# Last products on rows in block order, loaded inside the last expert block, and one-tile blocks with the rows stationary

## What is computed

```python
def reference(**kw):                          # cut to what matters, all fp32
    # 1. attention, 2 x 8 heads x 768 x 64: a window of +-15 keys and, beside it,
    #    24 summaries (max of k, mean of v over blocks of 32 keys), one softmax
    x = attn(q, k, v)                         # as rows [1536 tokens, 512]
    # 2. expert layer: each token goes to one of 8 experts
    logits = x @ w_gate
    expert_idx = argmax(logits, axis=1)
    gate_w = softmax(logits)[token, expert_idx]
    for e in range(8):                        # tokens of expert e
        out[mask] = gate_w[mask, None] * (relu(x[mask] @ w1[e]) @ w2[e])   # 512 -> 1024 -> 512
    # 3. dense layer, leaky relu
    h = out @ w_in                            # 512 -> 2048
    return maximum(0.01 * h, h) @ w_out       # 2048 -> 512
```

## Time and profile before

| | |
|---|---|
| median of 3 runs | 562.81 us (562.48 to 565.88) |
| the profiled execution | 563.63 us, of which the span from first to last instruction 561.9 us |
| mean granted TensorE clock | 0.987 of full |
| TensorE busy | 530.7 us, 94% of the span |
| VectorE / ScalarE / GpSimd busy | 53% / 48% / 14% |
| chain of work that ended last | TensorE 80%, VectorE 5%, ScalarE 5%, DMA 4% |
| HBM | 68.3 MB read, 11.3 MB written |

### The profile page before, as it was taken

One profiled execution on the slowest core, in us unless ns is written; L12 is line 12 of the kernel. 1 busy time (PEld: TensorE's weight loads), 2 busy tenths in 40 slices (PEclk: granted clock), 3 DMA queues, 4 the chain that ended last, 5 costly groups with the idle time before them and its releaser, 6 DMA issues.

```text
span 561.9 us, 9620 instructions
## 1 busy us (share of the span) xinstructions
PE 530.7 (94%) x3309; PEld 439.5 (78%) x3310; DVE 299.6 (53%) x575; ACT 267.7 (48%) x569; POOL 81.1 (14%) x123
## 2 busy tenths in 40 slices
PE   4899998979999999998869999999999999999997
PEld 3477777877888888898758888888888888888885
DVE  2678787774345245187715624754723763742631
ACT  4388778524344244378615525623633641642520
POOL 6127503014301310233200000000000000000000
PEclk9999999998999999999879999999999999999999
DMA  9999569028604524357770243144064052340001
GB/s 214 216 239 239 140 201 324 20 86 326 224 22 169 207 73 168 120 190 255 274 262 0 89 164 123 49 152 174 0 224 149 0 187 67 119 149 0 0 19 56
DMA packets 77964, 79.96 MB, mean 142 GB/s; under 512 B 45552, under 2 KB 47600, under 8 KB 77936
## 3 DMA queue, kind: packets, MB, share of 16 engines
q1 hardware_dynamic: 73168, 66.48, 38.7%
q0 software_dynamic: 3040, 9.96, 5.4%
q10 hardware_dynamic: 1728, 3.15, 1.5%
HBM read 68.30 MB, written 11.27 MB: 142 GB/s over the span
## 4 chain that ended last, share of the span: by engine, by line
PE 80%; DVE 5%; ACT 5%; DMA 4%; issue 3%; POOL 1%; SPq 0%; POOLq 0%; ACTq 0%; DVEq 0%
PE psum L1364 12%; PE psum L1365 12%; PE psum L1366 12%; PE psum L1382 11%; PE psum L1383 11%; PE psum L1384 11%; PE psum L1291 2%; PE psum L1224 2%; ACT p_sb L671 1%; PE psum L1279 1%; DMA y_rows<-y_sb,home_idx 1%; PE psum L1215 1%; PE psum L1180 1%; PE psum L1262 1%; PE psum L1199 1%
## 5 line engine op out<-in xcount | busy, mean ns | idle before, releaser
L1364 PE MATMUL psum<-xT_hi,w_hi 128*128 128x512 f32 (+2 forms) x352 | 130.2, 370 | 2.2 <-DVE w_lo L891 1.4
L1365 PE MATMUL psum<-xT_lo,w_hi 128*128 128x512 f32 (+2 forms) x352 | 129.0, 367 | 0.0
L1366 PE MATMUL psum<-xT_hi,w_lo 128*128 128x512 f32 (+2 forms) x352 | 128.9, 366 | 0.0
L1382 PE MATMUL psum<-w_hi,h_hi 128*128 128x512 f32 x296 | 116.9, 395 | 0.1
L1383 PE MATMUL psum<-w_lo,h_hi 128*128 128x512 f32 x296 | 116.0, 392 | 0.0
L1384 PE MATMUL psum<-w_hi,h_lo 128*128 128x512 f32 x296 | 115.8, 391 | 0.0
L891 DVE TENSOR_TENSOR w_lo<-w_raw,w_hi 128x512 fp32r<-128x512 f32 x88 | 57.0, 687 | 61.9 <-ACT w_hi L700 61.9
L1364 PEld LDWEIGHTS psum<-xT_hi,w_hi 128*128 128x128 f32 x352 | 66.7, 190 | 13.2 <-DVE xT_lo L901 2.8
L1366 PEld LDWEIGHTS psum<-xT_hi,w_lo 128*128 128x128 f32 x352 | 66.7, 190 | 10.2
L1365 PEld LDWEIGHTS psum<-xT_lo,w_hi 128*128 128x128 f32 x352 | 66.8, 190 | 10.0
L747 ACT ACTIVATE h_small<-psum 128x512 f32<-128x512 f32 x48 | 28.7, 598 | 89.8 <-PE psum L1366 89.8
(11 more groups left out here) (182 smaller groups left out, 535.6 us busy)
## 6 DMA issues: line engine op xcount, KB each, us to landing
w_raw<-in_moe_w_in SPq DMA_DIRECT2D x12, 1024.0 KB, 6.5
w_raw<-in_moe_w_out SPq DMA_DIRECT2D x6, 2048.0 KB, 8.5
w_raw<-in_moe_w SPq DMA_DIRECT2D x10, 1024.0 KB, 6.2
w_raw<-in_moe_w SPq DMA_DIRECT2D x5, 2048.0 KB, 8.3
q_nat<-in_q SPq DMA_DIRECT2D x12, 256.0 KB, 4.6
x_rows<-x_cur ACTq DMA_DIRECT2D x12, 256.0 KB, 3.8
x_rows_sb<-y_rows SPq DMA_DIRECT2D x12, 256.0 KB, 8.3
result<-y_sb SPq DMA_DIRECT2D x12, 256.0 KB, 2.0
```

Source lines behind the costliest of these rows:

```text
L1364: mm(h, w1_hi[:, c, cols], xT_hi[:, c, 0:n], start=(c == 0), stop=False)
L1365: mm(h, w1_hi[:, c, cols], xT_lo[:, c, 0:n], start=False, stop=False)
L1366: last = mm(h, w1_lo[:, c, cols], xT_hi[:, c, 0:n], start=False, stop=(c == KD - 1))
L1382: mm(y_ps[s % 2], h_hi[:, c, rows], w2_hi[:, c, :], start=(c == 0), stop=False)
```

## The change

1. The expert layer's results go to `y_dram` not at their token's row but at a "seat": block 1's rows first, then the later blocks' without the padding between them, and block 0's at the end. A column is added to `y_sb`, `x_rows` and `y_dram` (513 values a row) that carries the token's number. Padding rows go behind the 1536 real ones.
2. The first 512 seats are full when block 3 is stored. SP loads them inside block 4, and TensorE transposes them in two halves around the middle and the end of tile 0 of block 4's second product. The fill matmuls and the extra transposes go.
3. The gates are stored to DRAM once and fetched for each group of 512 by token number; each output tile is scattered by GpSimd to its tokens' rows.
4. A block of one tile runs its first product the other way round: the 128 rows stationary, 512 columns of w1 streaming, 2 x 4 x 3 = 24 matmuls. The hidden rows pass the relu, are transposed (8 transposes) and split after that.
5. In block 0: ScalarE makes the last w1 high parts together, GpSimd the four low parts of the upper half; VectorE makes slots, marks and plan in another order, with three w2 splits behind them; TensorE's inversion also waits for the plan. SP loads block 1's weights ahead of its loop.

The core of the diff (declarations, constants and repeated slices left out):

```diff
@@ SP
-            with sp.Fori(0, MAXB) as j:
+            next_e = sp.value_load(plan[0:1, 1:2], min_val=0, max_val=E - 1)
+            sp.wait_ge(w1_lo_ready, KF)
+            load_w1(next_e)
+            sp.wait_ge(w2_lo_ready, KF)
+            load_w2(next_e)
+            with sp.Fori(1, MAXB) as j:
...
                     with sp.If(n_blocks < j + 2):
-                        load_half(0, j + 1)
...
+                        load_half_w1(0, j + 1)
+                        sp.wait_ge(rows_transposed, KD * (j + 1))
+                        sp.sem_inc(sp_wait_over, 1)
+                        sp.wait_ge(y_stored, 16 * (SUB * j - (SUB - SUB0)))
+                        sp.sem_inc(sp_wait_over, 1)
+                        load_rows(0)
+                        load_half_w2(0, j + 1)
...
             sp.wait_ge(y_stored, 16 * (SUB * n_later + SUB0))
-            load_rows(0)
-            sp.sem_inc(y_out_free, 1)
...
-                for s in range(SUB):
-                    sp.wait_ge(y_ready, (u + 1) * SUB + s + 1)
-                    sp.dma_start(out[ds(g * ROWS + s * P, P), :], y_sb[:, s, :]).then_inc(out_stored, 16)
@@ GpSimd
+            pool.wait_ge(w1_lo_ready, KD)
+            for c in range(KD):
+                part = slice(F // 2, F)
+                pool.wait_ge(w1_hi_ready, KD + c + 1)
+                tt(w1_lo[:, c, part], w1_raw[:, c, part], w1_hi[:, c, part].bitcast(F32),
+                   ALU.subtract).then_inc(w1_lo_ready, 1)
...
+            def keep_ids(g):
+                for s in range(SUB):
+                    pool.wait_ge(rows_loaded[s], 16 * (g + 1))
+                nc.gpsimd.tensor_copy(out_idx[:, g, :], x_rows[:, :, DM].bitcast(I32)).then_inc(out_idx_ready, 1)
+                pool.wait_ge(out_idx_ready, g + 1)
+            def gather_gates(g):
+                if g:
+                    pool.wait_ge(y_ready, SUB * (n_blocks + HALVES * g))
+                    pool.sem_inc(out_wait_over, 1)
+                for s in range(SUB):
+                    pool.indirect_dma_start(
+                        out=row_gate[:, s:s + 1], out_offset=None, in_=gate_dram[:, :],
+                        in_offset=bass.IndirectOffsetOnAxis(ap=out_idx[:, g, s:s + 1].bitcast(U32), axis=0),
+                    ).then_inc(row_gate_ready, 16)
...
+            for g in range(GROUPS):
+                if g + 1 < GROUPS:
+                    keep_ids(g + 1)
+                for s in range(SUB):
+                    pool.wait_ge(y_ready, SUB * (n_blocks + HALVES * g + 1) + s + 1)
+                    pool.sem_inc(out_wait_over, 1)
+                    pool.indirect_dma_start(
+                        out=out[:, :], out_offset=bass.IndirectOffsetOnAxis(ap=out_idx[:, g, s:s + 1].bitcast(U32), axis=0),
+                        in_=y_sb[:, s, 0:DM], in_offset=None,
+                    ).then_inc(out_stored, 16)
+                if g + 1 < GROUPS:
+                    gather_gates(g + 1)
@@ ScalarE
+            def relu_tile(u):
+                for f in range(KD):
+                    split_w2(u, f)
+                for i in range(2):
+                    act.wait_ge(h_done, KF * u + 2 * i + 2)
+                    nc.scalar.activation(h_full[:, i, :], h_ps[i], ACT.Relu).then_inc(h_hi_ready, 2)
+                    for f in range(KD + 2 * i, KD + 2 * i + 2):
+                        split_w2(u, f)
+            def round_tile(u):
+                for i in range(2):
+                    act.wait_ge(h_done, KF * u + KD + 2 * i + 2)
+                    nc.scalar.copy(h_hi[:, KD * i:KD * i + KD, 0:P],
+                                   h_ps[2 + i].rearrange("p (f t) -> p f t", t=P)).then_inc(h_hi_ready, 2)
...
+                    used = act.value_load(used_tiles[0:1, ds(j, 1)], min_val=1, max_val=SUB)
@@ VectorE, block 0
             for f in range(KF):
                 rest_of_relu(0, f, ROWS0)
-                split_w2(0, f)
-                if W1_LEFT + f < KF:
-                    split_w1(0, W1_LEFT + f)
+                if f < 5:
+                    split_w2(0, f)
...
                 if f == 5:
-                    later_experts()
+                    dve.wait_ge(places_done, 2)
                     later_slots()
-                if f == 6:
                     slot_parts(T)
                     hot_tiles(T, LATER_TILES)
-            hot_rows(T)
+                if f == 6:
+                    hot_rows(T)
+                    later_experts()
+            for f in range(5, KF):
+                split_w2(0, f)
+            shift_logits()
+            later_tables()
             keep_gates()
-            later_tables()
@@ TensorE
-            def keep_busy(count):
-            def transpose_loaded_rows():
+            def first_of_tile(u, x):
+                for i in range(2):
+                    cols = slice(i * ROWS, (i + 1) * ROWS)
+                    for c in range(KD):
+                        pe.wait_ge(w1_lo_ready, 8 * u + KD * i + c + 1)
+                        if i == 0:
+                            pe.wait_ge(xT_lo_ready, KD * x + c + 1)
+                        mm(h_ps[i], xT_hi[:, c, 0:P], w1_hi[:, c, cols], start=(c == 0), stop=False)
+                        mm(h_ps[i], xT_hi[:, c, 0:P], w1_lo[:, c, cols], start=False, stop=False)
+                        last = mm(h_ps[i], xT_lo[:, c, 0:P], w1_hi[:, c, cols], start=False, stop=(c == KD - 1))
+                    last.then_inc(h_done, 2)
+            def transpose_hidden(u):
+                for i in range(2):
+                    pe.wait_ge(h_hi_ready, KF * u + 2 * i + 2)
+                    for f in range(KF // 2):
+                        last = nc.tensor.transpose(h_ps[2 + i][:, f * P:(f + 1) * P], h_full[:, i, f * P:(f + 1) * P], ident[:])
+                    last.then_inc(h_done, 2)
...
+            pe.wait_ge(experts_ready, 2)
             invert(inv_ps, T, LATER_TILES)
...
                     with pe.If(j + 1 < n_blocks):
                         transpose_rows(j + 1, rows_gathered, j + 2, 0, 2)
-                    second_product(j, 0, 1)
+                    with pe.If(used < 2):
+                        transpose_hidden(j)
+                    second_part(j, 0, 0, KF // 2)
+                    with pe.If(n_blocks < j + 2):
+                        transpose_rows(j + 1, rows_loaded, 1, 0, 2, 0)
+                    second_part(j, 0, KF // 2, KF)
```

More of the change, by code:

```diff
@@ L125, in build @@
         spare_row = keep("spare_row", [P, SLOT_TILES])
+        first_seat = keep("first_seat", [P, SUB0])
+        later_seat = keep("later_seat", [P, MAXB - 1, SUB])
+        padding = keep("padding", [E, P])
+        shift = keep("shift", [P, MAXB - 1, 1])
+        behind_pad = keep("behind_pad", [P, MAXB - 1, E])
         start_rows = keep("start_rows", [E, T, E], BF16)
@@ L159, in build @@
         used_f = keep("used_f", [1, MAXB - 1, 1])
-        ends = keep("ends", [1, 1, E])
-        behind = keep("behind", [1, MAXB - 1, E])
+        behind = keep("behind", [P, MAXB - 1, E])
         expert_f = keep("expert_f", [1, MAXB - 1, 1])
@@ L324, in build @@
         y_out_free = sem("y_out_free")
+        out_wait_over = sem("out_wait_over")
         def piece(m):
@@ L638, in _ @@
                     scatter(j)
+            def keep_ids(g):
[12 more added lines that the diff above has]
+                    ).then_inc(row_gate_ready, 16)
+            keep_ids(0)
+            pool.wait_ge(gate_stored, 16)
+            gather_gates(0)
+            n_later = pool.value_load(plan[0:1, MAXB + 1:MAXB + 2], min_val=1, max_val=MAXB - 1)
+            pool.wait_ge(y_stored, 16 * (SUB * n_later + SUB0))
+            pool.sem_inc(y_out_free, 1)
+            for g in range(GROUPS):
+                if g + 1 < GROUPS:
+                    keep_ids(g + 1)
+                for s in range(SUB):
+                    pool.wait_ge(y_ready, SUB * (n_blocks + HALVES * g + 1) + s + 1)
[6 more added lines that the diff above has]
+                    gather_gates(g + 1)
+                pool.wait_ge(out_stored, 16 * SUB * (g + 1))
+                pool.sem_inc(y_out_free, 1)
         @block.scalar
@@ L760, in second_product @@
                         split_w1(next_u, 2 * s + 1)
+                    if rows is not None:
+                        split_rows(rows, 0, 2)
                     if evacuate:
@@ L992, in count_blocks @@
                 last.then_inc(blocks_ready, 1)
+                dve.wait_ge(blocks_ready, 1)
+                stt(out=padding[:], in0=blocks[:], scalar=-float(ROWS), in1=total_ps,
+                    op0=ALU.mult, op1=ALU.add).then_inc(padding_ready, 1)
             def later_experts():
                 dve.wait_ge(places_done, 2)
-                chain(tt(behind[:], ends_ps.to_broadcast([1, MAXB - 1, E]),
-                         iota_tile[0:1, 0:MAXB - 1].unsqueeze(2).to_broadcast([1, MAXB - 1, E]), ALU.is_le))
-                chain(nc.vector.reduce_sum(expert_f[:, :, 0], behind[:], AX_X))
```

(22 more changed lines are left out.)

146 lines of the change are left out of this document (86 added, 60 removed).

## The result

The changed kernel takes 576.84 us in the median (575.67 to 578.67, 4 runs), the kernel before 563.22 beside it (4 runs). The ratio is 1.0211, 95% interval 1.0161 to 1.0261. The forecast was 558.3, range 551.5 to 565: wrong in sign. The profiled execution took 575.67, span 573.9, which is 12.0 us over the span before.

What follows compares the result with a forecast made beforehand. TensorE never waits in the long middle; gains lie in one-tile blocks and the open seam. Terms 2.0 + 3.7 - 2.1 - 9.95 + 1.8 = -4.55 take 563.63 to 559.1, less 0.8 for the median: 558.3, range 551.5 to 565.

Steps and rivals of the forecast that it cites:

- Block 3's gather: In block 3, gather of block 4's rows shares DMA with the earlier w2 load: +0.6 us, bounds 0 to +2.
- The rule on completion: A DMA's completion follows its engine's earlier writes; so block 4's gather, issued ahead of w2, would take 0.6 us less.
- Row length: Stored and loaded rows grow from 2048 to 2052 B; no cost taken.
- the rule on splitting: Runs off a 256 B multiple fetch up to 8 beats more on 64; under 1 us at the seam.
- a slow seam: Rival: row loads (+5.5) and scatter (+2.3) at the seam are slow, time 566.1; chance 0.13.
- The clock in block 3: In block 3, TensorE's idle of 7 us brings a clock dip: +1.2 us, bounds 0 to 1.7.
- Seam: From block 4's second product to the last stage's second hidden tile: 16.65 us, before 26.6, so -9.95.
- Tail: At the end, last rows leave by GpSimd's indirect DMA instead of SP's plain one: +1.8 us, bounds +0.7 to +3.
- the front: To the start of block 1: gather +0.5 and clock dip +1.6, +2.0 us, bounds -1 to +3.
- block 4: To its second product, ScalarE sets the pace: 11.4 us instead of 13.5, -2.1, bounds -4 and 0.
- the two full blocks: Middle blocks change nothing: products stand back to back, with the splits beside them.
- the last stage: After the second hidden tile, 266 us of the same dense work; its feeding has several us of slack per group.

Runs made afterwards that it cites:

- e1: Changed kernel, but SP loads the next block's second weights only after the block's last row gather has landed; ratio 1.0117.
- e3: Changed kernel, with one-tile blocks running the first product in the old 256-column form; ratio 1.0063.
- e6: Changed kernel with x_rows_sb and y_sb allocated at 528 columns a row in SBUF instead of 513; ratio 1.0207.
- e12: Kernel before, with y_rows in DRAM and y_sb at 513 columns, all 513 scattered and 512 loaded; ratio 1.0043.
- e9: Changed kernel with rows of 528 columns (2112 bytes) in DRAM and SBUF, the id written sixteen times behind each row; ratio 1.0143.
- e10: Changed kernel with 2112-byte rows and the next w2 load held until the last gather has landed; ratio 1.0100.
- e2: Changed kernel, with TensorE's block loop over the 4 later blocks this input has instead of all 10 possible; ratio 1.0154.
- e5: Kernel before, with GpSimd made to wait until the last output tile but one group is stored, then write one element; ratio 1.0080.
- e13: Changed kernel, with the wait for the last group's output stores moved from GpSimd to SP; ratio 1.0169.
- e7: Kernel before, with x_rows_sb alone allocated at 513 columns a row instead of 512; ratio 1.0132.
- e15: Kernel before with x_rows_sb of 513 columns, allocated behind xT_hi and h_small so that these do not move; ratio 1.0025.
- e4: Changed kernel with block 0 in its old order and no splits on GpSimd; ratio 1.0191.
- e8: Changed kernel with 528-column SBUF pitch, one-tile blocks in the 256-column form and TensorE's loop ended after block 4; ratio 1.0021.
- e14: Changed kernel with 2112-byte rows, 256-column form, TensorE's loop ended after block 4, and the last store wait moved to SP; ratio 0.9966.
- e11: Changed kernel with 2112-byte rows, one-tile blocks in the 256-column form and TensorE's loop ended after block 4; ratio 0.9997.

## Why the prediction was wrong

- **Block 3's gather, +0.6 with bounds 0 to 2, is the step that failed**: the wait ended 18.2 us after the block's first product instead of 12.25, so +6.0: 0.45 by later issue, the rest by the fourth gather's landing, 10.2 us for 4.7. I saw that the gather would be what is late, and that the w2 load moves up beside it (forecast 244.4, issued at 245.54), but had no row for a load issued behind a gather and took 0.6 us for it. e1 shows 2.9 us of it, the rows' length is 1.6 to 1.9, and 1.1 stays open. The rule on completion, by which the gather would not suffer, speaks only of the order in which completions are written; the same page of the Trainium skill (DMA: Bandwidth & Descriptors, Queues, rings and completion order) also says that each DMA engine takes turns between its queues packet by packet. The trace agrees as far as a load issued later does slow a gather issued earlier (10.2 against 7.3 us, e1); the third gather, in flight beside the same load, took 7.6 against 7.4.
- **Row length, priced at nothing.** I looked for its cost in the odd rows' own transfers, as the rule on splitting in the Trainium skill (DMA: Bandwidth & Descriptors, How a descriptor splits into AXI transactions) has it, and named a slow seam as the rival. (Its 8 beats on 64 are an eighth, not the seventh that I wrote.) The row loads at the seam took 4.1 us in the median against 3.5 before, but with the same rows 3.4 in e3 and 3.3 in e6, and e12, which reads 2048 bytes out of each row of 2052, took 3.5: nothing pins the 0.6 us on the rows. The pairs around e9 show it elsewhere, on gathers issued behind the scatter: 1.6 to 1.9 us in block 3.
- **The clock in block 3**, +1.2: from the gather's end to block 4's first product took 13.0 us, before 7.4; +5.6 where +3.1 was forecast (1.9 and 1.2). The second product started at half speed and reached full speed at 264.3, and cost 2.0 us more than before, the rows' transposes 0.9; the hidden transposes and their handover took 2.6. In e10, with 8.2 us of waiting, the second product ran at full speed and the same stretch took 11.1 (254.88 to 265.95). But the length of the wait alone does not set the dip: behind 10.7 us in e9 the second product ran at full speed (5.6 us), behind 9.8 in e1 it took 7.3.
- **Seam, -9.95**: came out at -5.35. Its first links were right: SP's loads went out 7.2 us after the last scatter's issue (forecast 6.9), SP loaded rows 1.2 us after block 4's second product began (1.75). Wrong were the loop's exit (3.0 us more between the transposes and the product, which e2 takes away, for 0.75 of waiting on VectorE), the row loads (6.45 us for 5.3; the rows of before give 5.1) and the clock in the first hidden tile (4.4 for 3.45). The exit stood in the timeline before, 2.25 us put down to "issue"; I took it away together with the fill products behind it.
- **Tail, +1.8 with bounds 0.7 to 3**: +6.2. I counted two ways to store a tile. They came to +1.1 (4.83 us from the last product to GpSimd's closing, before 3.75 to SyncE's at 561.67). What I left out is that the engine that waits for the last store must also close: the other 5.1. e5 gives 3.0 us for that alone, e13 gets 1.9 back; why the closing is 5.14 us here and not 3.2 is open.
- **Right**: the front (+1.0, in +2.0 with bounds -1 to 3, the gather and the dip as described), block 4 (-1.4 for -2.1, ScalarE setting the pace), the two full blocks, and the last stage, whose feeding cost nothing (261.78 against 261.77). The front's number is partly luck: in single traces block 3 starts at 236.1 to 240.5 us with the old front (e5, e7, e12, e15) and at 237.4 to 242.4 with the new, so that 1 us can't be told there, and e4's ratio can't tell it either.

The terms that failed are 7.9, 4.6 and 4.4 us. Block order and early rows save nearly what they were counted for once the loop's exit is gone: 9.0 us at the seam in e8, which is 4.7 us ahead at the last product. The rows-stationary form of one-tile blocks was the wrong part to count on. It shortened TensorE's work in a block whose length the gather sets, pulled the weight load onto that gather, and let the clock fall; e3 puts it at 1.5%, with an uncertainty of some 0.6.

## What to carry to other kernels

When an edit turns covered time into a wait, price that wait anew with everything the edit moves beside it, the loads released earlier above all: a landing time read behind cover is no price for one on the path. Ask of the last instruction on every engine what follows it, and whether it was covered before. A few bytes more per row should be tried at a padded pitch before the idea is judged.

## What was unexpected of the hardware

- GpSimd's closing instruction takes 3.2 us in the kernel before (at 283.8), in e7, e12 and e15, and 3.3 in e5, with no transfer of its own for 280 us. It takes 5.1 in the changed kernel and in every kernel made from it, counted in e13 and e14 from the end of the last scatter's issue. SyncE's takes 7 ns. The Trainium skill (VectorE: DVE Perf Modes, The DRAIN you can't avoid) gives some 12 ns for the drains in the instructions that the runtime adds around a kernel, on all five engines; the trace files GpSimd's under the kernel's own line, and that figure is no price for it. What makes it longer in the changed kernels was not tried. A scatter ahead of it alone does not, since in the kernel before one is issued at 281.24.
- Scattering rows of 2052 bytes slows the gathers behind them, though they read another tensor: the fourth of block 3 lands in 10.3 us against 8.3 with rows of 2112 bytes (e6, e9), and in 7.2 against 6.0 (e8, e11). Rows of 2112 bytes do not start on multiples of 256 either, three in four of them. Why was not tried.
- A tile of TensorE's operand placed 16 bytes further on in SBUF makes three products take 0.70 us instead of 0.68, 3.9 us over the last stage (e7, e15).
- Six empty turns of TensorE's dynamic loop hold up the products behind it by 2.9 us (e2), some 0.5 us each.
